# Second products of token tiles 1 and 3 one pair behind those of tiles 0 and 2 in a windowed mix, ELU and MLP kernel

## The chip, the cores and the metric

One core of one Trainium2 chip. The metric is the device time of one execution in microseconds, the median of several runs; beside it stands one profiled execution, from which all rows come. TensorE's granted clock is 1.0 at 2.4 GHz and 0.5 at 1.2 GHz.

## The reference

```python
w = softmax(weight_gen, axis=-1)            # (4, 4096, 8 heads, 7 taps)
x_unf = x_pad[:, idx, :].reshape(B, S, 7, 8, 24)
mixed = np.einsum('bshk,bskhg->bshg', w, x_unf)    # causal window of 7 tokens, d_model 192
h = mixed.reshape(16384, 192) @ w_in               # d_ff 2048
g = np.where(h > 0.0, h, np.exp(np.minimum(h, 0.0)) - 1.0)
out = g @ w_out                                    # (16384, 192)
```

The lines are the reference's in a shortened form; the softmax adds 1e-9 to its sum. All data is fp32.

## The kernel before, in words

Each of the 128 partitions holds a run of 128 consecutive tokens. A **block** is 4 tokens of each partition, that is 4 **token tiles** of 128 tokens, 512 tokens in all; there are 32 blocks. For each block:

- GpSimd makes the mix: `products` (L451, seven taps at once), `pair_sums` (L458), `last_sums` (L464, the last of them writes `mixed`), and for the softmax of a later block `shifted`, `guarded` and `scaled`. VectorE does the softmax's `max`, `sum` and `rec` (L553), ScalarE its exponential.
- VectorE turns `mixed` in 32x32 pieces (`turn`, L778); SP's queue sends it to DRAM and back as `x_raw`; ScalarE rounds it to `xt` (`high_parts`, L630) and GpSimd subtracts for `xt_lo` (`low_parts`, L485). This is done a block ahead.
- The matrix products run on fp32r values in high and low parts. d_ff is cut into 16 chunks, in 8 **pairs**. For a pair TensorE makes the **first products** (`half_products`, L866: high by high, low by high, high by low, 36 matmuls of 64 rows and 512 columns, two halves side by side) into two PSUM slots of four, then the **second products** of the pair before it in four steps (`second_products`, L878). A step takes two of the four accumulators (one PSUM bank for each token tile), half of the rows into one and half into the other: tiles (0, 2), (1, 3), (2, 0), (3, 1). Each step has 4 high matmuls of 384 columns (`g_hi` by `w_out` high and low together) and 4 low ones of 192 columns (`g_lo`).
- Between them lies the ELU: ScalarE `em = exp(h)` and `em - 1`, VectorE `max(min(em, 0), h)` back into the slot (L807), ScalarE `g_hi` (L658), VectorE `g_lo = slot - g_hi` (L813). That is the plain form, for pairs 0 to 3. Pairs 4 to 7 (`low_first`) treat the second chunk first and otherwise: VectorE `min(h, 0)` (L796), ScalarE exp, VectorE add -1 and max (L801). That is one operation fewer on ScalarE and one more on VectorE; it is called the longer form here.

All order is written out by hand: each engine's program is a list of pairs with waits on semaphores, and each engine works strictly in its order. TensorE's order is: first products of pair m + 1, second products of pair m; in pair 7 the first products are those of the next block's pair 0. At the start of a block VectorE must empty the four accumulators of the block before (`outputs`, L786, one reduction over high and low for each tile, in the order 2, 0, 3, 1) before TensorE may start the second products of pair 0 in them; `s_out` counts these reductions, `s_row` the halves of steps that TensorE has done, `s_split` the `g_lo`, `s_ghi` the `g_hi`. The four buffers for `g_hi` and `g_lo` hold two pairs.

```python
                for step, (j, products) in enumerate(steps):
                    if m == 0 and step < 2:
                        ge(pe, s_out, b.count(TILES, 2 * step + 2 - TILES))
                    ge(pe, s_row, b.count(STEPS, 2 * TILES * m + 2 * step - 2))
```

In block 0 the weights are also split: ScalarE rounds a quarter of `w_in` or `w_out` (`hi_half`, L596), VectorE subtracts (`low_half`, L750; its line is L756 where it reads a copy in PSUM, L760 where both inputs are in SBUF). Five of the eight quarters are done between the pairs, by `SPLIT_AT`: behind pair 0 `out` 1, pair 1 `in` 2, pair 2 `out` 2, pair 3 `in` 3, pair 4 `out` 3. They are called the first to the fifth split. `turn` stands ahead of pair 4 in block 0, of pair 3 in block 1, of pair 2 in all others.

## Time and profile before

| what | before |
|---|---|
| median of 3 runs | 1230.33 us (1230.3 to 1230.64) |
| profiled execution, its time | 1231.57 us |
| its span, first to last instruction | 1229.7 us |
| granted TensorE clock, mean | 0.991 |
| busy: TensorE, VectorE, ScalarE, GpSimd | 93%, 75%, 73%, 65% |
| DMA engines, mean over the span | 72 GB/s |

The profiled execution's own time is 1.87 us above its span; differences in the span are compared with that execution. In a timeline row stand the start and the length in us, the engine, the line, the operation with the tile that it writes and those that it reads, how many of them are merged into the row, and in brackets the idle time ahead of it with what ended that. PE is TensorE, PEld its weight loads, DVE VectorE, ACT ScalarE, POOL GpSimd. TensorE's merged rows overlap a little, so starts are compared with starts.

### The profile page before, as it was taken

The page shows a single profiled execution, that of the slowest core. Times are in us where ns is not written, and L with a number is a line of the kernel's source. Part 1 is how long each engine was busy: PE and PEld are TensorE (multiplying, and loading weights), DVE is VectorE, ACT ScalarE, POOL GpSimd, SP SyncE. Part 2 cuts the span into 40 slices and gives each one's busy share as a digit, 9 for nine tenths or more (in the row PEclk, how much of TensorE's full clock was granted, in tenths as well). Part 3 has the DMA queues.
Part 4 walks back from the last instruction along what each step waited for, and adds up shares of the span by engine and source line. Part 5 has one row for each costly group of instructions (what it writes and reads, how often), then busy time and mean ns, then how long its engine had stood idle before and what let it go on. Part 6 is the DMA issues. An engine that isn't in the chain of part 4 may idle for free.

```text
span 1229.7 us, 32008 instructions
## 1 busy us (share of the span) xinstructions
PE 1146.7 (93%) x12848; PEld 1021.8 (83%) x12848; DVE 921.1 (75%) x1431; ACT 900.0 (73%) x1549; POOL 802.4 (65%) x355
## 2 busy tenths in 40 slices
PE   4589999999999999999999999999999999999998
PEld 4478888888888888888888888888888888988887
DVE  7957777777777777777777777777777777777776
ACT  4457777777777777777777777777777777777775
POOL 7775667866667876667876667776667776667410
PEclk9889999999999999999999999999999999999999
DMA  7121333211232211223211233211323311331100
GB/s 217 44 74 40 89 88 88 86 55 33 87 87 87 84 57 33 87 87 87 87 56 31 87 87 87 87 59 30 87 87 87 87 60 31 83 87 51 52 14 14
DMA packets 58774, 88.02 MB, mean 72 GB/s; under 512 B 5224, under 2 KB 38500, under 8 KB 58720
## 3 DMA queue, kind: packets, MB, share of 16 engines
q1 hardware_dynamic: 58720, 87.42, 24.9%
q8 instruction: 19, 0.31, 0.1%
q14 instruction: 35, 0.29, 0.1%
HBM read 62.63 MB, written 24.77 MB: 71 GB/s over the span
## 4 chain that ended last, share of the span: by engine, by line
PE 78%; DVE 10%; ACT 5%; issue 5%; POOL 2%; DMA 0%; DVEq 0%; SPq 0%; POOLq 0%
PE acc L897 40%; PE slot L873 37%; DVE outs L789 5%; DVE g_lo L813 3%; ACT em L642 3%; ACT em L652 2%; POOL prod L453 1%; DMA xwin<-in_x_dram 0%; DVE slot L807 0%; DVE win_lo L760 0%; DVE wout L760 0%; POOL xt_lo L489 0%; POOL prod L470 0%; POOL prod L469 0%; DVE acc L730 0%
## 5 line engine op out<-in xcount | busy, mean ns | idle before, releaser
L897 PE MATMUL acc<-wout,g_hi 64*128 64x384 f32 x4096 | 548.6, 345 | 18.3 <-issue 12.0
L897 PE MATMUL acc<-wout,g_lo 64*128 64x192 f32 x4096 | 380.7, 264 | 44.8 <-DVE g_lo L813 44.4
L897 PEld LDWEIGHTS acc<-wout,g_lo 64*128 64x128 f32 x4096 | 367.0, 186 | 64.0 <-DVE g_lo L813 62.2
L807 DVE SCALAR_TENSOR_TENSOR slot<-em,slot 128x512 f32<-128x512 f32 x384 | 266.3, 695 | 185.9 <-ACT em L652 185.6
L642 ACT ACTIVATE em<-slot 128x512 f32<-128x512 f32 x384 | 227.3, 592 | 205.5 <-PE slot L873 205.5
L897 PEld LDWEIGHTS acc<-wout,g_hi 64*128 64x128 f32 x4096 | 328.7, 188 | 46.0 <-issue 24.4
L489 POOL TENSOR_TENSOR xt_lo<-x_raw,xt 128x512 fp32r<-128x512 f32 x93 | 118.8, 1292 | 358.3 <-ACT xt L635 358.3
L813 DVE TENSOR_TENSOR g_lo<-slot,g_hi 128x512 fp32r<-128x512 f32 x512 | 346.6, 689 | 5.3
L658 ACT ACTIVATE g_hi<-slot 128x512 fp32r<-128x512 f32 x512 | 304.8, 595 | 59.8 <-DVE slot L807 33.9
L453 POOL TENSOR_TENSOR prod<-xwin,probs 128x5376 f32<-128x5376 f32 (+1 forms) x32 | 305.9, 9559 | 7.1 <-POOL probs L448 5.4
L652 ACT ACTIVATE em<-em 128x512 f32<-128x512 f32 x384 | 242.7, 632 | 12.2
L873 PE MATMUL slot<-xt,win_hi 64*128 64x512 f32 (+1 forms) x1548 | 227.3, 399 | 2.6 <-ACT xt L592 1.3
L873 PE MATMUL slot<-xt,win_lo 64*128 64x512 f32 (+1 forms) x1548 | 221.6, 391 | 0.0
L873 PE MATMUL slot<-xt_lo,win_hi 64*128 64x512 f32 (+1 forms) x1548 | 217.8, 386 | 0.0
L873 PEld LDWEIGHTS slot<-xt,win_lo 64*128 64x128 f32 x1548 | 146.3, 186 | 33.6
L873 PEld LDWEIGHTS slot<-xt_lo,win_hi 64*128 64x128 f32 x1548 | 146.0, 186 | 32.2
L461 POOL TENSOR_TENSOR prod<-prod 128x2304 f32<-128x2304 f32 (+1 forms) x32 | 163.6, 5112 | 0.1
L801 DVE SCALAR_TENSOR_TENSOR slot<-em,slot 128x512 f32<-128x512 f32 x128 | 89.1, 696 | 89.8 <-ACT em L647 89.8
L873 PEld LDWEIGHTS slot<-xt,win_hi 64*128 64x128 f32 x1548 | 127.4, 188 | 14.4 <-POOL xt_lo L489 1.4
L647 ACT ACTIVATE em<-em 128x512 f32<-128x512 f32 x128 | 80.9, 632 | 32.3 <-DVE em L796 32.3
L796 DVE TENSOR_SCALAR em<-slot 128x512 f32<-128x512 f32 x128 | 88.5, 691 | 11.7 <-PE slot L873 10.4
L789 DVE TENSOR_REDUCE outs<-acc 128x192 f32<-128x384 f32 x128 | 62.2, 548 | 1.8 <-PE acc L897 1.8
(54 smaller groups left out, 406.2 us busy)
## 6 DMA issues: line engine op xcount, KB each, us to landing
xwin<-in_x_dram SPq DMA_DIRECT2D x29, 960.0 KB, 5.0
x_raw<-turned_dram SPq DMA_DIRECT2D x62, 384.0 KB, 4.7
out_dram<-outs SPq DMA_DIRECT2D x32, 384.0 KB, 2.6
turned_dram<-turned SPq DMA_DIRECT2D x124, 96.0 KB, 2.0
wg<-in_weight_gen_dram SPq DMA_DIRECT2D x32, 112.0 KB, 2.5
xwin<-in_x_dram SPq DMA_DIRECT2D x2, 768.0 KB, 4.6
win_raw<-in_moe_w_in_dram SPq DMA_DIRECT2D x24, 64.0 KB, 3.2
wout_raw<-in_moe_w_out_dram SPq DMA_DIRECT2D x4, 384.0 KB, 4.1
```

The lines of the kernel that those rows point to most:

```text
L453: done = nc.gpsimd.tensor_tensor(prod_of(first, end), taps_of(q, first, end), weights_of(q, first, end), ALU.mult)
L461: nc.gpsimd.tensor_tensor(prod[:, 0:half, first_tile * d_model:], prod[:, 0:half, first_tile * d_model:], prod[:, half:2 * half, first_til ...
L489: nc.gpsimd.tensor_tensor(by_tile(xt_lo[:, parity, k, :]), by_quad(x_raw[:, k, :]), by_tile(xt[:, parity, k, :].bitcast(F32)), ALU.subtrac ...
L642: nc.scalar.activation(em[:, f % 2, :], slot[slot_of(f)], ACT.Exp).then_inc(s_exp, 1)
L652: nc.scalar.activation(em[:, f % 2, :], em[:, f % 2, :], ACT.Copy, bias=-1.0).then_inc(s_em, 1)
L658: nc.scalar.activation(g_hi[:, f % GBUFS, :], slot[slot_of(f)], ACT.Copy).then_inc(s_ghi, 1)
L789: nc.vector.tensor_reduce(outs[:, parity, t, :], acc[t][:, 0:2 * d_model].rearrange("p (k d) -> p d k", k=2), AX.X, ALU.add).then_inc(s_ou ...
L801: nc.vector.scalar_tensor_tensor(out=slot[slot_of(f)], in0=em[:, 1, :], scalar=-1.0, in1=slot[slot_of(f)], op0=ALU.add, op1=ALU.max).then_ ...
L807: nc.vector.scalar_tensor_tensor(out=slot[slot_of(f)], in0=em[:, f % 2, :], scalar=0.0, in1=slot[slot_of(f)], op0=ALU.min, op1=ALU.max).th ...
L813: nc.vector.tensor_tensor(g_lo[:, f % GBUFS, :], slot[slot_of(f)], g_hi[:, f % GBUFS, :].bitcast(F32), ALU.subtract).then_inc(s_split, 1)
L873: last = pe.matmul(slot[slot_of(2 * m + h)][:, tokens], w[rows, k, cols], v[rows, parity, k, tokens], start=(n == 0), stop=(n == PASSES - 1))
L897: last = pe.matmul(acc[t][:, cols], g[rows, f % GBUFS, chunk(t)], wout[rows, f, 0:cols.stop - cols.start], start=(f == 0 and g is g_hi and ...
```

## The change

1. TensorE's second products are taken apart into tile pairs `EVEN` (tiles 0 and 2) and `ODD` (tiles 1 and 3). In the place of pair m's second products stand now: first odd step of pair m - 1, first even step of pair m, second odd step of pair m - 1, second even step of pair m. In pair 0 the pair before is pair 7 of the block before; the odd steps of the very last pair stand behind everything.
2. The outputs come in two groups: tiles 2 and 0 in pair 0 between its `max` and `g_lo`; tile 3 behind the first `max` of pair 1 and tile 1 behind the second. TensorE waits for the first group ahead of the first even step of pair 0 and for the second ahead of the first odd step that clears accumulators 1 and 3, in the place of pair 1.
3. Pair 0 gets the longer form. A `g_hi` buffer is free with the third step behind its pair instead of its own last.
4. TensorE waits for `xt` and `xt_lo` piece by piece instead of for all of `xt_lo`.
5. In blocks 0 and 1: `products` of block 1 are 8 instructions and its `pair_sums` 4; each of the five splits stands on VectorE ahead of the next pair instead of behind its own; `turn` in block 0 stands ahead of pair 5 instead of 4; steps of the softmaxes move by one or more pairs, and the `rec` for block 3 from pair 0 of block 1 to pair 3.

```diff
-    LOWS = PAIRS // 2
+    LOWS = PAIRS // 2 + 1
...
-            return block.count(STEPS, 2 * TILES * done)
+            return block.count(STEPS, 2 * TILES * done + 2)
...
-            return m >= PAIRS // 2
+            return m == 0 or m >= PAIRS // 2
...
+        LAST_ROW = {t: BLOCKS * STEPS - n for t, n in {2: 5, 0: 4, 3: 1, 1: 0}.items()}
...
-        DONE = (2, 0, 3, 1)
+        EVEN = ((0, 2), (2, 0))
+        ODD = ((1, 3), (3, 1))
+
+        def finished(b, t):
+
+            return b.count(STEPS, {2: STEPS - 5, 0: STEPS - 4, 3: STEPS + 1, 1: STEPS + 2}[t] - STEPS)
...
-            def pair_sums(b, first_tile=0):
+            def pair_sums(b, first_tile=0, pieces=1):
 
                 pool.wait_ge(s_prod, b.count(1, 1))
-                nc.gpsimd.tensor_tensor(prod[:, 0:half, first_tile * d_model:], prod[:, 0:half, first_tile * d_model:],
-                                        prod[:, half:2 * half, first_tile * d_model:], ALU.add).then_inc(s_add, 1)
+                each = (TILES - first_tile) // pieces * d_model
+                for at in range(first_tile * d_model, TILES * d_model, each):
+                    done = nc.gpsimd.tensor_tensor(prod[:, 0:half, at:at + each], prod[:, 0:half, at:at + each],
+                                                   prod[:, half:2 * half, at:at + each], ALU.add)
+                done.then_inc(s_add, 1)
...
-            products(1, 0, TILES)
+            for t in range(TILES):
+                for taps in ((0, BANK_TAPS), (BANK_TAPS, kernel)):
+                    done = nc.gpsimd.tensor_tensor(prod_of(t, t + 1)[:, taps[0]:taps[1]], taps_of(1, t, t + 1, taps),
+                                                   weights_of(1, t, t + 1, taps), ALU.mult)
+            done.then_inc(s_prod, 1)
...
-                return {("max", 0): 2, ("exp", 1): 2, ("sum", 1): 2, ("rec", 3): 2,
-                        ("max", 5): 3, ("exp", 7): 3, ("sum", 7): 3}
-            late = 6 if b.has_old else 7
+                return {("max", 0): 2, ("exp", 2): 2, ("sum", 2): 2, ("rec", 4): 2, ("max", 6): 3}
+            late = 7 if number(b) == 1 else 6
             at = {("rec", 0): 2, ("max", 4): 3, ("exp", late): 3, ("sum", late): 3}
+            if number(b) == 1:
+                at = {("exp", 0): 2, ("sum", 1): 2, ("rec", 3): 2, ("max", 4): 3, ("exp", late): 3, ("sum", late): 3}
...
                     softmax_step("rec", m)
-                    if m == turn_at(b)[0] and b.has_next:
+                    if b.first and m - 1 in SPLIT_AT:
+                        low_half(*SPLIT_AT[m - 1])
+                    if m == turn_at(b) and b.has_next:
                         turn(b)
...
                         elu(b, one)
+                        if m == 0 and b.has_previous:
+
+                            dve.wait_ge(s_stored[1 - q], b.per_parity(16, 16 * q))
+                            output(b, 2, 1 - q)
+                            output(b, 0, 1 - q)
                         low(b, two)
                         low(b, one)
                     else:
                         elu(b, one)
+                        if m == 1 and b.has_previous:
+                            output(b, 3, 1 - q)
                         elu(b, two)
-                        if m == 0 and b.has_previous:
-
-                            dve.wait_ge(s_stored[1 - q], b.per_parity(16, 16 * q))
-                            outputs(b, 1, 1 - q)
+                        if m == 1 and b.has_previous:
+                            output(b, 1, 1 - q)
                         low(b, one)
                         low(b, two)
-                    if b.first and m in SPLIT_AT:
-                        low_half(*SPLIT_AT[m])
...
+                rows = 2 * TILES * m - TILES
+                if m == 0 and b.first:
+                    pe.wait_ge(s_ghi, 2)
+                    tiles_of(b, 0, EVEN[0], 0)
+                    tiles_of(b, 0, EVEN[1], 2)
+                    return
+                earlier = (b, m - 1) if m > 0 else (previous(b), PAIRS - 1)
+                if m == 1:
+
+                    ge(pe, s_out, b.count(TILES))
+                tiles_of(*earlier, ODD[0], b.count(STEPS, rows - 2))
+                if m == 0:
+                    pe.wait_ge(s_out, b.count(TILES, 2 - TILES))
+                pe.wait_ge(s_ghi, b.count(CHUNKS, 2 * m + 2))
+                tiles_of(b, m, EVEN[0], b.count(STEPS, rows))
+                tiles_of(*earlier, ODD[1], b.count(STEPS, rows + 2))
+                tiles_of(b, m, EVEN[1], b.count(STEPS, rows + 4))
```

VectorE at the start of a block (any but the first two), before: the two `max` of pair 0, the reductions, two `g_lo`, then pair 1.

```order
L566 RECIPROCAL wrec<-wsum 128x32 [waits s_psoft]
L807 SCALAR_TENSOR_TENSOR slot<-em,slot 128x512 [waits s_em] x2
L789 TENSOR_REDUCE outs<-acc 128x192 [waits s_row,s_stored1]
L789 TENSOR_REDUCE outs<-acc 128x192 [waits s_row] x3
L813 TENSOR_TENSOR g_lo<-slot,g_hi 128x512 [waits s_ghi] x2
L807 SCALAR_TENSOR_TENSOR slot<-em,slot 128x512 [waits s_em] x2
L813 TENSOR_TENSOR g_lo<-slot,g_hi 128x512 [waits s_ghi] x2
```

The same place now:

```order
L589 RECIPROCAL wrec<-wsum 128x32 [waits s_psoft]
L818 TENSOR_SCALAR em<-slot 128x512 [waits s_filled]
L823 SCALAR_TENSOR_TENSOR slot<-em,slot 128x512 [waits s_exp]
L829 SCALAR_TENSOR_TENSOR slot<-em,slot 128x512 [waits s_em]
L811 TENSOR_REDUCE outs<-acc 128x192 [waits s_row,s_stored1]
L811 TENSOR_REDUCE outs<-acc 128x192 [waits s_row]
L835 TENSOR_TENSOR g_lo<-slot,g_hi 128x512 [waits s_ghi] x2
L829 SCALAR_TENSOR_TENSOR slot<-em,slot 128x512 [waits s_em]
L811 TENSOR_REDUCE outs<-acc 128x192 [waits s_row]
L829 SCALAR_TENSOR_TENSOR slot<-em,slot 128x512 [waits s_em]
L811 TENSOR_REDUCE outs<-acc 128x192 [waits s_row]
L835 TENSOR_TENSOR g_lo<-slot,g_hi 128x512 [waits s_ghi] x2
```

Two reductions are ahead of the first two `g_lo` where four were, one operation (L818) came into pair 0, and the other two reductions stand in pair 1.

VectorE in block 0, before, from the end of pair 2 to L796 of pair 5; L760 are the third, fourth and fifth split:

```order
L760 TENSOR_TENSOR wout<-wout_raw,wout 128x4x192 [waits s_whi]
L566 RECIPROCAL wrec<-wsum 128x32 [waits s_psoft]
L807 SCALAR_TENSOR_TENSOR slot<-em,slot 128x512 [waits s_em] x2
L813 TENSOR_TENSOR g_lo<-slot,g_hi 128x512 [waits s_ghi] x2
L760 TENSOR_TENSOR win_lo<-win_raw,win_hi 128x3x256 [waits s_whi]
L783 STREAM_TRANSPOSE turned<-mixed 128x768 [waits s_add]
L796 TENSOR_SCALAR em<-slot 128x512 [waits s_filled]
L801 SCALAR_TENSOR_TENSOR slot<-em,slot 128x512 [waits s_exp]
L807 SCALAR_TENSOR_TENSOR slot<-em,slot 128x512 [waits s_em]
L813 TENSOR_TENSOR g_lo<-slot,g_hi 128x512 [waits s_ghi] x2
L760 TENSOR_TENSOR wout<-wout_raw,wout 128x4x192 [waits s_whi]
L796 TENSOR_SCALAR em<-slot 128x512 [waits s_filled]
```

The same place now:

```order
L585 TENSOR_REDUCE wsum<-probs 128x32 [waits s_esoft]
L782 TENSOR_TENSOR wout<-wout_raw,wout 128x4x192 [waits s_whi]
L829 SCALAR_TENSOR_TENSOR slot<-em,slot 128x512 [waits s_em] x2
L835 TENSOR_TENSOR g_lo<-slot,g_hi 128x512 [waits s_ghi] x2
L589 RECIPROCAL wrec<-wsum 128x32 [waits s_psoft]
L782 TENSOR_TENSOR win_lo<-win_raw,win_hi 128x3x256 [waits s_whi]
L818 TENSOR_SCALAR em<-slot 128x512 [waits s_filled]
L823 SCALAR_TENSOR_TENSOR slot<-em,slot 128x512 [waits s_exp]
L829 SCALAR_TENSOR_TENSOR slot<-em,slot 128x512 [waits s_em]
L835 TENSOR_TENSOR g_lo<-slot,g_hi 128x512 [waits s_ghi] x2
L782 TENSOR_TENSOR wout<-wout_raw,wout 128x4x192 [waits s_whi]
L805 STREAM_TRANSPOSE turned<-mixed 128x768 [waits s_add]
```

`turn` (the transpose) was ahead of pair 4 and is now ahead of pair 5, behind the fifth split; `rec` went from pair 3 to pair 4, `wsum` from pair 1 to the end of pair 2.

## Rows read from the trace of the kernel before

**Rows 1.** The page, part 1: busy time and share of each engine.

```profile
PE 1146.7 (93%) x12848; PEld 1021.8 (83%) x12848; DVE 921.1 (75%) x1431; ACT 900.0 (73%) x1549; POOL 802.4 (65%) x355
```

**Rows 2.** Waits from 119.97 to 1188.5: us in total, times, longest.

```profile
PE acc L897 <- DVE g_lo L813: 41.5, 29, 1.5
```

**Rows 3.** Timeline of TensorE around a block's start: start us, us, line, operation.

```profile
594.67 0.88 PE L873 MATMUL slot<-xt,win_hi 64*128 64x512 f32 x6
...
599.03 0.88 PE L873 MATMUL slot<-xt,win_hi 64*128 64x512 f32 x6
...
601.16 0.62 PE L897 MATMUL acc<-wout,g_hi 64*128 64x384 f32 x4
603.21 0.47 PE L897 MATMUL acc<-wout,g_lo 64*128 64x192 f32 x4 [1.43 <-DVE g_lo L813]
```

**Rows 4.** Timeline of VectorE at the same place.

```profile
600.01 1.94 DVE L789 TENSOR_REDUCE outs<-acc 128x192 f32<-128x384 f32 x4
601.88 1.28 DVE L813 TENSOR_TENSOR g_lo<-slot,g_hi 128x512 fp32r<-128x512 f32 x2
...
605.74 0.97 DVE L783 STREAM_TRANSPOSE turned<-mixed 128x768 f32<-128x768 f32 x1
```

**Rows 5.** Timeline of ScalarE and VectorE in a pair of the longer form.

```profile
1214.68 0.60 ACT L642 ACTIVATE em<-slot 128x512 f32<-128x512 f32 x1 [0.94 <-PE slot L873]
...
1216.83 1.26 ACT L658 ACTIVATE g_hi<-slot 128x512 fp32r<-128x512 f32 x2
...
1217.46 1.36 DVE L813 TENSOR_TENSOR g_lo<-slot,g_hi 128x512 fp32r<-128x512 f32 x2
```

**Rows 6.** Timeline of ScalarE, then of VectorE, in pair 0.

```profile
596.97 0.60 ACT L642 ACTIVATE em<-slot 128x512 f32<-128x512 f32 x1 [0.94 <-PE slot L873]
...
598.26 0.70 DVE L807 SCALAR_TENSOR_TENSOR slot<-em,slot 128x512 f32<-128x512 f32 x1 [1.26 <-ACT em L652]
599.41 0.69 DVE L807 SCALAR_TENSOR_TENSOR slot<-em,slot 128x512 f32<-128x512 f32 x1 [0.45 <-ACT em L652]
```

**Rows 7.** Timeline of VectorE, then of GpSimd, in block 0.

```profile
26.66 3.73 DVE L760 TENSOR_TENSOR wout<-wout_raw,wout 128x768 fp32r<-128x768 f32 x1
...
45.13 10.19 DVE L760 TENSOR_TENSOR win_lo<-win_raw,win_hi 128x768 fp32r<-128x768 f32 x1
...
60.23 0.96 DVE L760 TENSOR_TENSOR wout<-wout_raw,wout 128x768 fp32r<-128x768 f32 x1
61.10 0.68 DVE L796 TENSOR_SCALAR em<-slot 128x512 f32<-128x512 f32 x1
...
31.31 5.15 POOL L461 TENSOR_TENSOR prod<-prod 128x2304 f32<-128x2304 f32 x1
...
39.63 1.84 POOL L470 TENSOR_TENSOR prod<-prod 128x768 f32<-128x768 f32 x1
...
44.79 9.70 POOL L453 TENSOR_TENSOR prod<-xwin,probs 128x5376 f32<-128x5376 f32 x1 [0.27 <-POOL probs L448]
```

**Rows 8.** Timeline of three engines around block 1, and one window.

```profile
69.33 1.66 ACT L635 ACTIVATE xt<-x_raw 128x512 fp32r<-128x512 f32 x3
...
79.72 0.36 DVE L566 RECIPROCAL wrec<-wsum 128x32 f32<-128x32 f32 x1 [4.54 <-POOL wsum L441]
...
78.29 0.88 PE L873 MATMUL slot<-xt,win_hi 64*128 64x512 f32 x6
...
119.97 0.88 PE L873 MATMUL slot<-xt,win_hi 64*128 64x512 f32 x6
...
core 0: us, PE busy (x) PEld busy (x) DVE busy (x) ACT busy (x) POOL busy (x), PEclk, DMA share, GB/s
78.30:92.00 13.70, 10.51 (x82) 8.80 (x80) 7.07 (x13) 5.35 (x10) 13.38 (x7) 0.75 0.32 110
```

**Rows 9.** Timeline at the end: VectorE and TensorE.

```profile
1224.95 1.95 DVE L789 TENSOR_REDUCE outs<-acc 128x192 f32<-128x384 f32 x4 [1.77 <-PE acc L897]
1225.06 0.36 PE L897 MATMUL acc<-wout,g_lo 64*128 64x192 f32 x4
```

More of the change, by code:

```diff
@@ L243, in turn_at, with copies_at @@
         def turn_at(b):
-            return (4, (0, 3)) if b.first else (3, (0, 3)) if not b.has_old and b.pair == 0 else (2, (1, 2))
+            return 5 if b.first else 3 if number(b) == 1 else 2
+        def copies_at(b):
+            return {6: (0, PIECES)} if b.first else {5: (0, PIECES)} if number(b) == 1 else {4: (0, 1), 5: (1, PIECES)}
+        LAST_ROW = {t: BLOCKS * STEPS - n for t, n in {2: 5, 0: 4, 3: 1, 1: 0}.items()}
         def by_quad(t):
@@ L277, in taps_of, with weights_of @@
                            ap=[list(t.ap[0]), [d_model, taps[1] - taps[0]], [group, (end - first) * heads], [1, group]])
[L279 to L280 removed]
+        def weights_of(q, first, end, taps=(0, kernel)):
+            t = probs[:, q, first * HK + taps[0]:]
             return bass.AP(tensor=t.tensor, offset=t.offset,
[L282 removed]
+                           ap=[list(t.ap[0]), [1, taps[1] - taps[0]], [kernel, (end - first) * heads], [0, group]])
         def bank_weights(taps):
@@ L411, in _, with previous @@
                 sp.wait_ge(s_stored[q], 16 * (BLOCKS // 2 + 1))
+        def previous(b):
+            return Block(b.pair, 0) if b.parity == 1 else Block(b.pair - 1, 1)
         def following(b):
@@ L542, in body @@
                 sums(b)
-            sums(one_)
+            sums(one_, pieces=TILES)
             with pool.Fori(1, BLOCKS // 2 - 2) as pair:
@@ L656, in high @@
                 act.wait_ge(s_g, place(b, f))
-                ge(act, s_row, used_count(b, f - GBUFS))
+                if not (b.first and f < GBUFS):
+                    act.wait_ge(s_row, used_count(b, f - GBUFS))
                 nc.scalar.activation(g_hi[:, f % GBUFS, :], slot[slot_of(f)], ACT.Copy).then_inc(s_ghi, 1)
             def body(b):
-                at, pieces = turn_at(b)
                 softmax = softmaxes(b)
@@ L850, in _ @@
             unrolled_blocks(body)
-            b = Block(BLOCKS // 2 - 1, 1)
             dve.wait_ge(s_stored[1], 16 * (BLOCKS // 2))
-            outputs(b, 0, 1)
+            for t in (2, 0, 3, 1):
+                nc.vector.wait_ge(s_row, LAST_ROW[t])
+                nc.vector.tensor_reduce(outs[:, 1, t, :],
+                                        acc[t][:, 0:2 * d_model].rearrange("p (k d) -> p d k", k=2), AX.X,
+                                        ALU.add).then_inc(s_out, 1)
         @block_of.tensor
@@ L871, in half_products @@
                     w, v = ((win_hi, xt), (win_lo, xt), (win_hi, xt_lo))[n // PIECES]
+                    if m == 0 and copied is not None and n // PIECES == 0:
+                        pe.wait_ge(s_xthi, copied.count(PIECES, k + 1))
+                    if m == 0 and copied is not None and n // PIECES == 2:
+                        pe.wait_ge(s_xtlo, copied.count(PIECES, k + 1))
                     for h, rows in enumerate(HALVES):
@@ L882, in second_products @@
                 lo = (g_lo, slice(d_model, 2 * d_model))
-                highs, lows_ = ((one, hi), (two, hi)), ((one, lo), (two, lo))
-                steps = [(j, highs + lows_) for j in range(TILES)]
-                pe.wait_ge(s_ghi, b.count(CHUNKS, two + 1))
-                for step, (j, products) in enumerate(steps):
-                    if m == 0 and step < 2:
-                        ge(pe, s_out, b.count(TILES, 2 * step + 2 - TILES))
-                    ge(pe, s_row, b.count(STEPS, 2 * TILES * m + 2 * step - 2))
-                    for n, (f, (g, cols)) in enumerate(products):
-                        if j == 0 and f == one and g is g_lo:
-                            pe.wait_ge(s_split, b.count(CHUNKS, two + 1))
-                        for h, rows in enumerate(HALVES):
-                            t = (j + 2 * h) % TILES
-                            last = pe.matmul(acc[t][:, cols], g[rows, f % GBUFS, chunk(t)],
-                                             wout[rows, f, 0:cols.stop - cols.start],
-                                             start=(f == 0 and g is g_hi and step < 2),
-                                             stop=(f == CHUNKS - 1 and g is g_lo and j >= 2))
-                            if n == len(products) - 1:
-                                last.then_inc(s_row, 1)
@@ new lines, in tiles_of @@
+                ge(pe, s_row, rows_done)
+                for n, (f, (g, cols)) in enumerate(((one, hi), (two, hi), (one, lo), (two, lo))):
+                    if n == 2 and tiles == EVEN[0]:
+                        pe.wait_ge(s_split, b.count(CHUNKS, two + 1))
+                    for t, rows in zip(tiles, HALVES):
+                        last = pe.matmul(acc[t][:, cols], g[rows, f % GBUFS, chunk(t)],
+                                         wout[rows, f, 0:cols.stop - cols.start],
+                                         start=(f == 0 and g is g_hi and tiles in (EVEN[0], ODD[0])),
+                                         stop=(f == CHUNKS - 1 and g is g_lo and tiles in (EVEN[1], ODD[1])))
+                        if n == 3:
+                            last.then_inc(s_row, 1)
```

37 lines of the change are left out of this document (17 added, 20 removed).

## The prediction

> **What bounds the kernel now.** I read the page first. The reader is to see TensorE busy for 93% of the span and no other engine above 75% [rows 1], so the question is where TensorE stands still. The list of waits answers for the 29 blocks from 120 to 1188.5 us: one wait counts there, 29 times for VectorE's `g_lo`, 41.5 us in all, 1.43 us a block [rows 2]. The timeline of TensorE at a block's start then shows the place [rows 3]. First products of a pair start at 594.67 and of the next at 599.03: a pair costs 4.36 us where nothing waits, of which the first products take 2.10 and the four steps of the second ones 2.26 (0.57 each). Eight pairs are 34.88 us. But a block takes (599.03 - 119.97) / 13 = 36.85 us [rows 3, 8], so 1.97 us are lost per block: 1.43 in that wait, the rest in the restart around it (0.28 before 601.16) and one later pair. VectorE's rows give the reason [rows 4]: from 600.01 it reduces all four accumulators (0.49 us each, start to start), and only then subtracts the two `g_lo`, 601.88 to 603.16; TensorE's low products start at 603.21.
>
> Below, T is the start of the first products of pair 1 (599.03), and F the moment when a pair's two slots are full; at a block's start F = T - 2.08 (ScalarE's exponential, 596.97, starts 0.02 after F [rows 6]).
>
> **The change, part by part.**
>
> *TensorE's order.* No product is added or removed in a block. In the second products of pair 0 TensorE now first does a step of the pair before, so the first `g_lo` is wanted later: 2.10 (first products) + 0.57 (odd step) + 0.35 (high part) = T + 3.02, instead of T + 2.45.
>
> *VectorE and ScalarE in pair 0.* It now takes the form of pairs 4 to 7. VectorE gets one operation more (0.69 us), ScalarE one fewer (0.63). Such a pair, measured: slots full at 1214.66, the two `g_lo` start at 1217.46 when the second `max` ends, so F + 2.80, and end 1.35 later [rows 5]. With two reductions (2 x 0.485 = 0.97) between: F + 5.12 = T + 3.04, and 0.04 to reach TensorE: T + 3.08. Against T + 3.02 a wait of 0.06 is left, and a product that starts after a wait costs 0.11 more than in the stream (0.47 against 0.36 us [rows 3]). I take **0.17 us left per block, so 1.80 saved**. Bounds: 1.97 (nothing left) and 1.2 (VectorE comes 0.6 late to pair 0).
>
> *Pair 1.* The plain form: `max` of the first chunk starts at F + 1.32 and of the second at F + 2.47 [rows 6]. F is T + 2.10. Tile 3 is finished by the third step of pair 0, T + 2.1 + 1.7 + some 0.2 = T + 4.0 to 4.1; VectorE is ready for it at T + 4.1. Then reduction, `max`, reduction, two `g_lo`: T + 7.2. TensorE wants them at T + 6.46 + 0.57 + 0.35 = T + 7.38, and the cleared accumulators at T + 6.46, when VectorE is done with them at T + 5.8. Nothing waits; the slack is 0.2.
>
> *Behind it.* `turn` starts at T + 7.15 in place of T + 6.71 [rows 4]. Its two transfers and ScalarE's first copy, at T + 18.6, have 1.7 us of slack left. On SP's queue the store of the outputs, and the loads of weights and of the window behind it, go out some 3 us later, but are wanted 15 us later at the earliest. A g_hi buffer is now free with the third step of the following pair, F + 1.7 to 1.9; ScalarE asks for it at F + 2.17 [rows 5]. All this costs nothing; the cover is 0.3 us in the last case.
>
> *The start, blocks 0 and 1.* VectorE's splitting of weights (both inputs in SBUF) takes 0.96 us at 60.23, but 3.73 and 10.19 at 26.66 and 45.13 [rows 7]. The second ends 0.8 us after GpSimd's products, 44.79 + 9.70 [rows 7]: while GpSimd runs one long instruction, this operation waits. Now the products and first sums of block 1 are in 12 pieces (a quarter of 5.15 is 1.3, an eighth of the products 1.0 to 1.4), the splits stand one place later, and `turn` behind the last of them.
>
> Followed with these durations, VectorE: pair 0 (now of the longer form) through at 22.1 + 4.15 = 26.2; first split waits for a piece, through near 28.1 instead of 30.4; pair 1 until 30.8; second split 32.2; pair 2 and the `wsum` behind it 36.3; third split, behind a piece, 38.2; pair 3 until 40.9 instead of 45.1; fourth split behind one of the last sums (1.84 [rows 7]), 43.7; pair 4 (4.15), 47.8. GpSimd: products 19.9 to 31.1 (8 pieces, a split between them), first sums with two splits between until 38.9, `wsum` 0.3, three sums of 1.84 and a split 6.5, scaling 0.8: products of block 2 from 46.4 to 56.1 instead of 44.8 to 54.5. So the fourth split, which waited 9.2 us, goes free, but VectorE comes to the fifth at 47.8, 1.4 us after those products began, and it waits until 57. `turn` follows, pair 5 begins at 57.9 instead of 61.10 [rows 7]: 3.2 us gained, but `turn` ends at 57.9 instead of 56.2. ScalarE copied x 13.1 us after `turn`'s end, when its pair 6 was through [rows 8]; the data needs 9.1 (last transfer issued at 60.9, landing 4.4 to 4.7 later), so the copies now start at 67.0, the last `xt_lo` is there at 71.5, pair 7 at 72.7. The first products of block 1 no longer wait for the last `xt_lo`: T of block 1 comes at about 74.2 instead of 78.29 [rows 8], **4.1 us**. In block 1 before, VectorE stood 4.54 us for GpSimd's `wsum` [rows 8], TensorE's granted clock was 0.75 over the 13.7 us behind (1.2 GHz for half of them), and the block took 119.97 - 78.29 = 41.68. `rec` has moved to pair 3, so block 1 should take 34.88 + 0.5 (pair 0) + 1.2 (`turn` in pair 3 waits for `mixed`) = 36.6: **5.1 us**. Together 9.2. Bounds: 5 (the pieces give nothing) and 18 (the last split comes before the products).
>
> The Trainium skill (SBUF — State Buffer, Who interferes with whom) says that a VectorE instruction with two SBUF inputs and a GpSimd one that reads SBUF block each other for a whole instruction, and that issue order decides who waits. The long split's row agrees on the first; no row here shows the order between two ready pieces. Read literally it speaks against this part, since GpSimd's next piece could be issued ahead of the split; the sum would then be 1171.6 (rival C).
>
> *The end.* TensorE has one odd step more behind the last wait (0.57) and a step that waits for the one before it (some 0.2). Four reductions from 1224.95, the first beside the last products of 1225.06 [rows 9], become two behind the end, which saves some 0.4: **0.4 us more**.
>
> **Sum**, against the profiled execution (span 1229.7, time 1231.57): 30 boundaries (into blocks 2 to 31) x 1.80 = 54.0; start 9.2; end -0.4: 62.8 us less, a span of 1166.9. The median of the runs is 1230.33, and the same difference gives **1167.5 us**.
>
> **Rivals.**
> (A) The forecast, its range 1160 to 1176, chance 0.62.
> (B) The boundary wait shrinks but stays: VectorE has the longer chain in pair 0, and any lateness goes one for one into TensorE's wait. For it: the margin is nil (-0.06). Against: VectorE ends a pair 0.2 before the next F (1218.82 against 1219.02 [rows 5]), and `rec` takes 0.34 of which only 0.05 is late. With 0.6 more per block: 18 us, 1185. Chance 0.14.
> (C) GpSimd's pieces let no split in until its queue waits for a semaphore. For it: its rows stand back to back, and no row shows a split between two ready pieces. Then the first 4.1 are lost: 1171.6. Chance 0.13. The page of the Trainium skill named above would have it so if its order of issue is that of the queues.
> (D) VectorE reaches the last split before the products of block 2 start; it is only 1.4 us late by my working. It then saves 8 of the 9.2 us that it waits: 1159. Chance 0.07.
> (E) Slower: each step of the second products waits for its accumulators' last step. If the new interleaving made it wait for the step directly ahead of it, as at the end, each of 1024 steps would pay a restart of 0.11 to 0.2 us. From 0.06 us per step that eats the gain of 62.8; at 0.11 it costs 113 us: 1280. Against: the counts waited for lie two steps back in both orders, and consecutive steps always use other banks. Chance 0.03.
> (F) The wait does not go because something else, late at the same place, ends it: no change but the start's. I give no change within 0.2% (about what a measurement of this kernel can tell) 0.01.
>
> **How the numbers follow.** The likeliest is A: 1167.5. The range 1158 to 1184 takes in A, C, D and most of B's bounds. Faster: A to D, 0.96; same 0.01; slower 0.03.
>
> **What would show it.** In the new profile TensorE's wait for `g_lo` at the low product should be under 0.2 us per block and the block period 35.0 to 35.1; VectorE's reductions should stand in two pairs, with a `max` between the later two and the first `g_lo` pair ending near T + 3.1. The last split should show some 9 us, the other splits under 2.5. Block 1's T near 74, block 2's near 111, with no stretch at a granted clock of 0.75 behind 78. A period above 35.4 would refute the pair-0 working, a T of block 1 above 77 the start's.

## The result, and the profile after

The changed kernel took 1159.7 us in the median of its first four runs, against 1230.32 for the kernel before in the same comparison: a ratio of 0.943, with a 95% interval of 0.9376 to 0.9484. The four runs were 1155.2, 1155.6, 1163.8 and 1165.6; two later sets gave 1165.2 (four runs, ratio 0.9469, 0.9455 to 0.9484) and 1166.1 (five runs, ratio 0.9474, 0.9461 to 0.9487). The forecast was 1167.5. So there are two groups of runs, near 1155 (two runs) and from 1163.8 to 1167.3 (eleven); the first median, 1159.7, lies between them, where no run does, and what follows on the profile is about the longer group. The profiled execution took 1163.79 us with a span of 1162.0, 67.7 less than before.

The page of the changed kernel: TensorE's busy share and the granted clock in 40 slices.

```profile
PE 1129.5 (97%) x12848; PEld 1027.8 (88%) x12848; DVE 926.4 (80%) x1463; ACT 882.1 (76%) x1517; POOL 806.5 (69%) x365
...
PEclk9989999999999999999999999999999999999999
```

TensorE is busy for 97% of the span instead of 93% [rows 1]. In the list of waits from 110 to 1115 us (us in total, times, longest) the line that answers to [rows 2]:

```profile
PE acc L922 <- DVE g_lo L835: 0.4, 1, 0.4
```

The wait that counted 29 times is left once, in block 2. TensorE at the block's start that answers to [rows 3]:

```profile
598.91 0.88 PE L907 MATMUL slot<-xt,win_hi 64*128 64x512 f32 x6
...
601.55 0.53 PE L922 MATMUL acc<-wout,g_hi 64*128 64x384 f32 x4
601.92 0.36 PE L922 MATMUL acc<-wout,g_lo 64*128 64x192 f32 x4
...
603.27 0.88 PE L907 MATMUL slot<-xt,win_hi 64*128 64x512 f32 x6
```

T is 598.91. From T to the next first products are 4.36 us, as between any two pairs: the low product of 601.92 runs 0.37 behind the high one, 0.36 long, so nothing was waited for. VectorE in pairs 0 and 1 of the same block, answering to [rows 4, 6]:

```profile
596.88 0.69 DVE L818 TENSOR_SCALAR em<-slot 128x512 f32<-128x512 f32 x1
...
598.93 0.69 DVE L829 SCALAR_TENSOR_TENSOR slot<-em,slot 128x512 f32<-128x512 f32 x1
599.54 1.01 DVE L811 TENSOR_REDUCE outs<-acc 128x192 f32<-128x384 f32 x2
600.47 1.27 DVE L835 TENSOR_TENSOR g_lo<-slot,g_hi 128x512 fp32r<-128x512 f32 x2
...
603.11 0.55 DVE L811 TENSOR_REDUCE outs<-acc 128x192 f32<-128x384 f32 x1
603.65 0.70 DVE L829 SCALAR_TENSOR_TENSOR slot<-em,slot 128x512 f32<-128x512 f32 x1
604.25 0.55 DVE L811 TENSOR_REDUCE outs<-acc 128x192 f32<-128x384 f32 x1
604.72 1.28 DVE L835 TENSOR_TENSOR g_lo<-slot,g_hi 128x512 fp32r<-128x512 f32 x2
605.92 0.97 DVE L805 STREAM_TRANSPOSE turned<-mixed 128x768 f32<-128x768 f32 x1
```

Two reductions from 599.54, `g_lo` until 601.74, which is 0.18 before TensorE's low product; then a reduction on each side of the second `max` of pair 1 (603.65), and the transpose at T + 7.01. The span splits as follows; the T of blocks 1, 2 and 31 are starts of TensorE's first products:

```profile
73.13 0.88 PE L907 MATMUL slot<-xt,win_hi 64*128 64x512 f32 x6
...
108.93 0.88 PE L907 MATMUL slot<-xt,win_hi 64*128 64x512 f32 x6
...
1122.35 0.88 PE L907 MATMUL slot<-xt,win_hi 64*128 64x512 f32 x6
```

| stretch | before | after | difference | forecast |
|---|---|---|---|---|
| start to T of block 1 | 78.29 | 73.13 | -5.2 | -4.1 |
| block 1 | 41.68 | 35.80 | -5.9 | -5.1 |
| blocks 2 to 30 | 1068.6 | 1013.4 | -55.2 | -52.2 |
| block 31, to the last exponential | 30.4 | 28.5 | -2.0 | -1.8 |
| from there to the end | 10.7 | 11.2 | +0.5 | +0.4 |
| span | 1229.7 | 1162.0 | -67.7 | -62.8 |

The starts of 1188.6 and 1219.04 (before) and 1150.82 (after) come from the same timelines. VectorE and GpSimd in block 0, where L782 are the splits, answering to [rows 7]:

```profile
26.41 1.20 DVE L782 TENSOR_TENSOR wout<-wout_raw,wout 128x768 fp32r<-128x768 f32 x1
...
36.39 1.49 DVE L782 TENSOR_TENSOR wout<-wout_raw,wout 128x768 fp32r<-128x768 f32 x1
...
40.62 1.81 DVE L782 TENSOR_TENSOR win_lo<-win_raw,win_hi 128x768 fp32r<-128x768 f32 x1
...
46.49 8.98 DVE L782 TENSOR_TENSOR wout<-wout_raw,wout 128x768 fp32r<-128x768 f32 x1
55.39 0.96 DVE L805 STREAM_TRANSPOSE turned<-mixed 128x768 f32<-128x768 f32 x1
...
18.76 11.41 POOL L533 TENSOR_TENSOR prod<-xwin,probs 128x768 f32<-128x768 f32 x8
...
25.59 1.21 POOL L533 TENSOR_TENSOR prod<-xwin,probs 128x576 f32<-128x576 f32 x1
26.75 2.26 POOL L533 TENSOR_TENSOR prod<-xwin,probs 128x768 f32<-128x768 f32 x1
...
44.95 9.71 POOL L469 TENSOR_TENSOR prod<-xwin,probs 128x5376 f32<-128x5376 f32 x1 [0.27 <-POOL probs L464]
```

The rows of 25.59 and 26.75 are the sixth and seventh of the eight pieces in the row above them, taken by a narrower window. The first split, started at 26.41, took 1.20 us: it ended 0.81 behind the sixth piece, and the seventh took 2.26 us where its like took 1.54, so it was the seventh that waited. GpSimd's program has no wait between these pieces. The third split (1.49) got in between the last piece of the first sums and `wsum`, the fourth (1.81) waited for the second half of one of the last sums and went ahead of the next. The fifth was reached at 46.49, 1.5 us after the products of block 2 began, and took 8.98: it ended 0.8 behind them. TensorE's rows, and then a window, show what that costs, answering to [rows 8]:

```profile
59.67 1.01 PE L922 MATMUL acc<-wout,g_hi 64*128 64x384 f32 x4 [8.91 <-ACT g_hi L683]
...
63.07 1.42 PE L907 MATMUL slot<-xt,win_hi 64*128 64x512 f32 x6
```

```profile
core 0: us, PE busy (x) PEld busy (x) DVE busy (x) ACT busy (x) POOL busy (x), PEclk, DMA share, GB/s
50.00:73.00 23.00, 13.57 (x132) 12.10 (x132) 17.55 (x20) 11.44 (x20) 10.97 (x6) 0.78 0.22 52
```

TensorE stood 8.91 us and came back at 1.2 GHz: the six products at 63.07 take 1.42 us instead of 0.88; over the window the granted clock is 0.78. The stretch at 0.75 behind 78 is gone, as forecast: from 78 to 92 us the granted clock is 1.00. At T of block 2 stand VectorE's `rec` and two of TensorE's rows with what is left of the waits:

```profile
107.94 0.35 DVE L589 RECIPROCAL wrec<-wsum 128x32 f32<-128x32 f32 x1 [0.70 <-POOL wsum L457]
...
112.06 0.61 PE L922 MATMUL acc<-wout,g_hi 64*128 64x384 f32 x4 [0.32 <-DVE outs L811]
113.07 0.47 PE L922 MATMUL acc<-wout,g_lo 64*128 64x192 f32 x4 [0.40 <-DVE g_lo L835]
```

The end, answering to [rows 9]: TensorE's last odd step, and VectorE's last reductions, of which now only two stand behind it.

```profile
1157.27 0.62 PE L922 MATMUL acc<-wout,g_hi 64*128 64x384 f32 x4
...
1156.72 1.02 DVE L881 TENSOR_REDUCE outs<-acc 128x192 f32<-128x384 f32 x2 [1.76 <-PE acc L922]
1158.13 1.02 DVE L881 TENSOR_REDUCE outs<-acc 128x192 f32<-128x384 f32 x2 [0.39 <-PE acc L922]
```

### The profile page after: what moved, and what is told of

It is laid out like the page before. It is cut to its first block, busy times and chain, and to the rows that moved or that the text cites. A ratio compares the mean times of both kernels' runs of the same rounds, so it can differ in the third digit from the quotient of the medians.

```text
span 1162.0 us, 32004 instructions
## 1 busy us (share of the span) xinstructions
PE 1129.5 (97%) x12848; PEld 1027.8 (88%) x12848; DVE 926.4 (80%) x1463; ACT 882.1 (76%) x1517; POOL 806.5 (69%) x365
## 4 chain that ended last, share of the span: by engine, by line
PE 86%; POOL 7%; issue 2%; DVE 2%; DMA 1%; ACT 1%; SPq 0%; POOLq 0%; DVEq 0%
PE acc L922 45%; PE slot L907 42%; POOL prod L469 2%; POOL prod L479 2%; POOL prod L533 1%; DVE g_lo L835 1%; POOL xt_lo L508 1%; DMA turned_dram<-turned 0%; DMA x_raw<-turned_dram 0%; POOL prod L488 0%; POOL prod L489 0%; DVE slot L823 0%; DVE slot L829 0%; ACT em L671 0%; DVE outs L811 0%
## 5 line engine op out<-in xcount | busy, mean ns | idle before, releaser
L922 PE MATMUL acc<-wout,g_lo 64*128 64x192 f32 x4096 | 374.3, 260 | 0.8 <-DVE g_lo L835 0.4
L922 PEld LDWEIGHTS acc<-wout,g_lo 64*128 64x128 f32 x4096 | 371.0, 185 | 4.7 <-DVE g_lo L835 3.4
L666 ACT ACTIVATE em<-slot 128x512 f32<-128x512 f32 x352 | 208.5, 592 | 133.6 <-PE slot L907 133.6
L469 POOL TENSOR_TENSOR prod<-xwin,probs 128x5376 f32<-128x5376 f32 (+1 forms) x31 | 296.4, 9561 | 7.2 <-POOL probs L464 6.8
L676 ACT ACTIVATE em<-em 128x512 f32<-128x512 f32 x352 | 222.7, 633 | 11.2
L479 POOL TENSOR_TENSOR prod<-prod 128x2304 f32<-128x2304 f32 (+2 forms) x35 | 164.8, 4711 | 0.1
L818 DVE TENSOR_SCALAR em<-slot 128x512 f32<-128x512 f32 x160 | 109.4, 684 | 8.1 <-PE slot L907 7.9
L659 ACT ACTIVATE xt<-x_raw 128x512 fp32r<-128x512 f32 x93 | 54.8, 625 | 23.3 <-DMA x_raw<-turned_dram 23.1
```

The costliest lines, as they stand in the source:

```text
L469: done = nc.gpsimd.tensor_tensor(prod_of(first, end), taps_of(q, first, end), weights_of(q, first, end), ALU.mult)
L479: done = nc.gpsimd.tensor_tensor(prod[:, 0:half, at:at + each], prod[:, 0:half, at:at + each], prod[:, half:2 * half, at:at + each], ALU.add)
L666: nc.scalar.activation(em[:, f % 2, :], slot[slot_of(f)], ACT.Exp).then_inc(s_exp, 1)
L676: nc.scalar.activation(em[:, f % 2, :], em[:, f % 2, :], ACT.Copy, bias=-1.0).then_inc(s_em, 1)
L818: nc.vector.tensor_scalar_min(em[:, 1, :], slot[slot_of(f)], 0.0).then_inc(s_low, 1)
L922: last = pe.matmul(acc[t][:, cols], g[rows, f % GBUFS, chunk(t)], wout[rows, f, 0:cols.stop - cols.start], start=(f == 0 and g is g_hi and ...
```

## The experiments

T of block 1 and of block 2 and the period of the later blocks (the commonest distance of two T, to within 0.01 or 0.02) are from each kernel's profile. The three profiles of the changed kernel have T of block 1 up to 0.9 us apart, so a smaller difference there says nothing. All kernels ran beside the kernel before, which had medians of 1230.65, 1230.66 and 1231.16 us.

| kernel | median us | T of block 1 | T of block 2 | period |
|---|---|---|---|---|
| before | 1230.3 | 78.29 | 119.97 | 36.85 |
| changed (profiles of three sets) | 1159.7, 1165.2, 1166.1 | 73.13, 73.89, 74.00 | 108.93, 109.72, 109.82 | 34.88 |
| start_only | 1224.9 | 75.23 | 112.07 | 36.85 |
| longform_before | 1225.2 | 79.11 | 121.56 | 36.51 |
| whole | 1167.4 | 76.04 | 111.88 | 34.88 |
| gate | 1157.2 | 65.39 | 101.24 | 34.88 |
| gate_plain0 | 1165.0 | 66.26 | 102.16 | 35.21 |
| gate_extra | 1170.1 | 65.98 | 102.20 | 35.32 |
| gate_strict | 1157.2 | 66.08 | 101.87 | 34.88 |
| whole_x | 1161.6 | 70.17 | 106.00 | 34.88 |
| turn_first | 1156.6 | 64.94 | 100.78 | 34.88 |

**again, again2: the changed kernel, unaltered.**

> The changed kernel, unaltered. Its four runs so far were 1155.2, 1155.6, 1163.8 and 1165.6 us, with mean granted clocks of 0.998, 0.997, 0.993 and 0.992, so there are two groups some 9 us apart. Theory: they are two outcomes of block 0. In one VectorE's fifth split waits 9 us for GpSimd's products of block 2 (as in the profiled run, T of block 1 at 73.1), in the other it starts ahead of them and T comes some 8 us earlier, with no stretch at half clock near 60 us. Rival: the steady part differs, by a lowered clock somewhere behind 110 us. If the profile falls into the fast group, T of block 1 near 65 speaks for the theory, 73 for the rival.

> The changed kernel, unaltered, once more, since of eight runs two were 9 us shorter and no profile of such a run is at hand. Theory: in those VectorE's fifth split started ahead of GpSimd's products of block 2, as the gated kernel (1157.15) makes it do always; a profile in the fast group must then show that split at about 1 us and T of block 1 near 65. Rival: split at 9 us also in a fast profile, with the time gained elsewhere. If all runs are slow (1164 to 1166) it stays open.

All nine runs lay in the longer group: 1164.7 to 1165.6 and 1165.7 to 1167.3. There is no edit. Both profiles show the fifth split at 8.98 us. No profile of a run near 1155 was had, so what happened in the two of 13 stays open. Their mean granted clocks, 0.998 and 0.997, are those of the gated kernel below (0.996 to 0.999) and not those of the other eleven (0.992 to 0.994), which fits a missing stand of TensorE and does not show it; the next experiment shows that a deliberate early split gives about that time.

**gate: GpSimd starts the products of block 2 only when all splits are done.**

```diff
                 pool.wait_ge(s_add, b.count(ADDS))
+                pool.wait_ge(s_wlo, len(SPLITS))
                 products(q, 0, TILES)
```

> The changed kernel; GpSimd's products of block 2 (and of all later blocks, where it costs nothing) also wait until all eight splits are done. Theory (the fifth split's 9 us wait is what sets T of block 1): the split takes about 1 us, TensorE has no idle stretch of 9 us between 50 and 60, T of block 1 near 65 instead of 73.1, all runs in one group at 1153 to 1157 us. Rival (the transfers of x and GpSimd's later products hide it): T of block 1 stays at 71 to 73 and the runs at 1162 to 1166.

1157.15 us (1155.95 to 1157.6), ratio 0.9404 (0.9391 to 0.9417) to the kernel before, and 8.0 less than the changed kernel beside it. VectorE and GpSimd in its timeline, and a window of it:

```profile
46.63 0.96 DVE L783 TENSOR_TENSOR wout<-wout_raw,wout 128x768 fp32r<-128x768 f32 x1
...
47.73 9.73 POOL L469 TENSOR_TENSOR prod<-xwin,probs 128x5376 f32<-128x5376 f32 x1 [2.91 <-DVE wout L783]
```

```profile
50.00:73.00 23.00, 20.58 (x218) 17.00 (x216) 17.25 (x29) 16.53 (x30) 17.04 (x7) 1.00 0.25 61
```

The split takes 0.96 instead of 8.98 and GpSimd starts 2.8 later; the long stand of TensorE is gone and the clock stays at 1.00. T of block 1 is at 65.39, 8.5 earlier than in the changed kernel beside it. The theory of the fifth split holds, and this version is faster than the kernel before and than the longer group of the changed one.

**whole: products and first sums of block 1 as one instruction each.**

```diff
-            for t in range(TILES):
-                for taps in ((0, BANK_TAPS), (BANK_TAPS, kernel)):
...
+            products(1, 0, TILES)
...
-            sums(one_, pieces=TILES)
+            sums(one_)
```

> The changed kernel with products and first sums of block 1 in one instruction each again (12 pieces to 2). Theory: the first and third split wait for the long instructions, 2 to 4 us each, VectorE reaches the fifth split 3 to 5 us later, but that waits for the products of block 2 all the same, so T of block 1 stays within 1.5 us of 73.1: 1162 to 1167 us, and no run in the group near 1155. Rival (the pieces carry the gain at the start): 1168 us or more.

1167.4 against 1165.2 beside it: T of block 1 is 2.0 to 2.9 later. That is more than my 1.5, and the median lies just above my range and just below the rival's. Its VectorE and GpSimd:

```profile
32.27 3.79 DVE L778 TENSOR_TENSOR win_lo<-win_raw,win_hi 128x768 fp32r<-128x768 f32 x1
...
48.79 8.98 DVE L778 TENSOR_TENSOR wout<-wout_raw,wout 128x768 fp32r<-128x768 f32 x1
...
39.40 0.90 POOL L457 TENSOR_TENSOR wsum<-wsum,eps 128x32 f32<-128x32 f32 x1 [4.16 <-DVE wsum L581]
...
47.24 9.71 POOL L469 TENSOR_TENSOR prod<-xwin,probs 128x5376 f32<-128x5376 f32 x1 [0.27 <-POOL probs L464]
```

The first two splits take 3.16 and 3.79 us (I had named the first and third; the third took 0.95), so `wsum` comes late, GpSimd stands 4.16 for it, and the products of block 2 start at 47.24 instead of 44.95. The fifth split waits behind them as before. I had left out that the late splits hold GpSimd up through `wsum`.

**start_only: the start's part alone, on the kernel before.** Its edits are those of the change's fifth item, among them:

```diff
-                    if b.first and m in SPLIT_AT:
-                        low_half(*SPLIT_AT[m])
...
-            products(1, 0, TILES)
+            for t in range(TILES):
+                for taps in ((0, BANK_TAPS), (BANK_TAPS, kernel)):
...
-            sums(one_)
+            sums(one_, pieces=TILES)
```

> The kernel before with the start's part of the change alone (pieces, splits one place later, turn of block 0 at pair 5, softmax steps moved); TensorE's order, outputs and pair 0 as before. By the prediction's sum the start is worth 9.2 us of 62.8; the changed profile says 11.0 with all parts. Theory: 1219 to 1222 us, the block period still 36.85. Rival (the start gains only together with TensorE's new order): 1225 or more.

1224.9 us, 5.7 less, ratio 0.9957 (0.9942 to 0.9973), outside my 1219 to 1222 and just short of the rival. The profiled execution was the shortest of the four (1223.76 to 1225.79): its span is 7.8 less, T of block 2 is 7.9 earlier and the period unchanged. That is less than the 9.2 to 11 of the theory. TensorE's rows show what is missing:

```profile
70.78 0.96 PE L881 MATMUL slot<-xt,win_hi 64*128 64x512 f32 x6 [1.04 <-POOL xt_lo L492]
...
79.41 0.47 PE L905 MATMUL acc<-wout,g_lo 64*128 64x192 f32 x4 [1.46 <-DVE g_lo L821]
```

TensorE stands 1.04 us for all of `xt_lo` ahead of block 1, which the piecewise wait takes away, and the wait at the boundary, 1.46 us here, stays in block 1, which takes 36.84 us instead of 35.80. So the 11 us at the start of the changed kernel are 8 of this part and 3 of the others.

**whole_x: the gated kernel, TensorE waits for all of `xt_lo` again.**

```diff
                     elif b.has_next:
+                        pe.wait_ge(s_xtlo, b.count(PIECES, PIECES))
                         pe.wait_ge(s_split, b.count(CHUNKS, CHUNKS - 2))
-                        half_products(1 - q, 0, range(PASSES), copied=b)
+                        half_products(1 - q, 0, range(PASSES))
```

> The gated kernel in which TensorE again waits for all of xt_lo before the first products of the next block. Theory: in later blocks xt_lo is there long before (period stays 34.9), in block 0 the products start some 3 us later, of which 2.1 us are those that now run ahead of the last xt_lo: T of block 1 near 67.5 and 1159 to 1160 us. Rival (the piecewise wait is worth nothing): 1157.

1161.6 us, 4.4 more, T of block 1 at 70.17. TensorE's row of those products:

```profile
63.58 1.65 PE L908 MATMUL slot<-xt,win_hi 64*128 64x512 f32 x6 [4.91 <-POOL xt_lo L508]
```

They start 4.5 later than in the gated kernel (59.04), behind a stand of 4.91 us, and the first six of them take 1.65 us; the granted clock from 63 to 66 us is 0.50, where the gated kernel has 1.00. All 36 first products ran at half the clock: 4.01 us from 63.58 to the next second products, where they take 2.10 at the full one. The stand also cost the clock, which I had not counted; T of block 1 is 4.8 later and not 2.1. The later blocks do not change.

**turn_first: the gated kernel with `turn` ahead of the fifth split.**

```diff
-                    if b.first and m - 1 in SPLIT_AT:
-                        low_half(*SPLIT_AT[m - 1])
                     if m == turn_at(b) and b.has_next:
                         turn(b)
+                    if b.first and m - 1 in SPLIT_AT:
+                        low_half(*SPLIT_AT[m - 1])
```

> The gated kernel with turn ahead of the fifth split instead of behind it. Theory: in the gated kernel ScalarE's copies of x in block 0 wait 2.5 us for the transfers behind turn; turn ends 0.9 earlier, so do the copies, but GpSimd's products, which wait for the split, end 0.9 later and hold the first xt_lo: T of block 1 0 to 1 us earlier than 65.4, 1156 to 1157 us. Rival (turn alone counts): 1155 or less.

1156.6 us (1155.3 to 1157.4) against 1157.15 in another set: T of block 1 is 0.45 earlier, as the theory has it, but that is less than the 0.9 by which profiles of one kernel differ there, and the medians do not tell the two kernels apart. It stays open; the rival's 1155 or less did not come.

**longform_before: the kernel before with the longer form in pair 0.**

```diff
-            return m >= PAIRS // 2
+            return m == 0 or m >= PAIRS // 2
```

> The kernel before with only the longer form in pair 0 (TensorE's order, outputs and start as before). Theory: the second max of pair 0 ends 0.36 us earlier (F + 2.80 instead of F + 3.16), the four reductions and g_lo follow, so the wait for g_lo falls from 1.43 to about 1.1 us and the block period from 36.85 to 36.5: 30 x 0.36 = 11 us, 1219 to 1221 us. Rival (VectorE's added operation eats it): 1230 or more.

The period falls by 0.35 to 36.51, as computed; TensorE's wait there:

```profile
601.41 0.47 PE L897 MATMUL acc<-wout,g_lo 64*128 64x192 f32 x4 [1.22 <-DVE g_lo L813]
```

But the median is 1225.2, 5.5 less and not 11: T of block 3 comes 2.1 us later than before (158.90 against 156.84), so the first blocks give part of it back: block 0 0.8, block 1 0.8, block 2 0.5. In block 1 VectorE's `rec` stands 4.53 us for GpSimd's `wsum`, as before. Now L796 stands behind it and ScalarE's exponential waits for L796, so TensorE stands 3.11 us for `g_hi` in that block instead of 1.73.

**gate_plain0: the gated kernel with pair 0 in the plain form.** The first two reductions then stand behind its second `max`.

```diff
-            return m == 0 or m >= PAIRS // 2
+            return m >= PAIRS // 2
```

> The gated kernel (1157.15) with pair 0 in the plain form again. In the changed profile g_lo ends 2.83 us after T and is wanted at T + 3.01, so the slack is 0.18. Theory: the reductions and g_lo come 0.36 later, a wait of about 0.2 and a restart of 0.1 come back: block period 35.1 to 35.3, 1164 to 1170 us. Rival (TensorE's new order alone takes the wait away): period 34.88, 1157 us.

1165.0 us, period 35.21: 0.33 per block come back, and with them 7.9 us (the mean of blocks 2 to 30 is 35.22 instead of 34.94, 8.0 us in all). So, since start_only left the period where it was, whole_x did not change it and gate_strict shows the buffers' release to be free, TensorE's new order with outputs in two groups is worth 36.85 - 35.21 = 1.64 us per block and the longer form 0.33. The order and the two groups were not run apart.

**gate_extra: one more reduction in pair 0.**

```diff
+                            dve.wait_ge(s_row, finished(b, 2))
+                            nc.vector.tensor_reduce(spare[:], acc[2][:, 0:2 * d_model].rearrange("p (k d) -> p d k", k=2),
+                                                    AX.X, ALU.add)
                             output(b, 2, 1 - q)
```

> The gated kernel with one more reduction (into a spare tile) ahead of the two in pair 0 of every block but the first. Theory (the chain of VectorE in pair 0 has 0.18 us of slack and every further us goes into TensorE's wait): 0.485 - 0.18 + 0.1 = 0.4 us per block, period 35.3, 31 x 0.4 = 12.5 us: 1168 to 1171 us. Rival (more slack than the rows show, or a wait for something else): below 1160.

1170.1 us, period 35.32, 0.44 more. VectorE and TensorE at a block's start:

```profile
598.80 0.55 DVE L864 TENSOR_REDUCE spare<-acc 128x192 f32<-128x384 f32 x1
599.27 1.01 DVE L813 TENSOR_REDUCE outs<-acc 128x192 f32<-128x384 f32 x2
600.20 1.28 DVE L837 TENSOR_TENSOR g_lo<-slot,g_hi 128x512 fp32r<-128x512 f32 x2
...
601.53 0.47 PE L927 MATMUL acc<-wout,g_lo 64*128 64x192 f32 x4 [0.18 <-DVE g_lo L837]
```

The wait is back, 0.18 us idle and a product of 0.47 instead of 0.36. `g_lo` ends at 601.48 and the product starts at 601.53, so of the 0.18 us between `g_lo` and the product in the changed kernel 0.05 are the way to TensorE and 0.13 are slack. My estimates with 0.13 come out at both ends: 0.485 - 0.13 + 0.11 = 0.46 here (measured 0.44) and 0.36 - 0.13 + 0.11 = 0.34 in gate_plain0 (measured 0.33). The chain of VectorE in pair 0 is the next limit.

**gate_strict: g_hi buffers free a step later.**

```diff
-            return block.count(STEPS, 2 * TILES * done + 2)
+            return block.count(STEPS, 2 * TILES * done + 4)
```

> The gated kernel in which ScalarE waits for a g_hi buffer until the fourth instead of the third step behind its pair. The third step ends at about F + 1.9 and ScalarE asks at F + 2.17 (cover 0.3), the fourth at F + 2.45. Theory: g_hi comes up to 0.3 us later in pairs of the longer form, but TensorE wants it only at F + 4.9 and g_lo at F + 5.3 (they come at F + 3.4 and 4.2): period 34.9, 1157 to 1158 us. Rival (the buffers' release is the next limit): 0.3 per pair, 8 pairs, 31 blocks: over 1200 us.

1157.2 us, period 34.88. Its waits (whole run):

```profile
ACT g_hi L684 <- PE acc L923: 34.2, 123, 1.0
...
PE acc L923 <- DVE g_lo L836: 0.6, 2, 0.4
```

ScalarE now waits 34.2 us in 123 places (in the gated kernel 0.4 in one), and the period does not show it.

## Why the prediction was right

*The wait at the block's start: right, its rest too large.* I had the pair's `g_lo` end at F + 5.12, 0.06 us too late, and left 0.17 per block. It ends at F + 4.92 (601.74, with F at 596.82), 0.18 ahead of its product, and in most blocks nothing is left: they take 34.88. The mean of blocks 2 to 30 is 34.95, with block 2 at 36.08; without it 34.91. The term that was mis-sized is "F + 5.12", 0.20 too much. I began the reductions where the second `max` ends, but they start 0.08 before that (599.54, with the `max` from 598.93 for 0.69); I took 0.97 for two reductions, but `g_lo` starts 0.93 behind the first (600.47); and the two `g_lo` take 1.27 behind a reduction instead of 1.35 behind a `max`. The rows of the kernel before had it: reductions at 600.01 under a `max` that ends at 600.10 [rows 4, 6] and 1.28 for the two `g_lo` behind them [rows 4]. Blocks 3 to 30 gave 4.1 us more than forecast and block 2 took 1.0 back, so 3 of the 4.9 us between forecast and measured span lie here. gate_extra and gate_plain0 bear out the margin; rival B, a wait that shrinks but stays, is what those two kernels have, and single blocks of the changed one (last section).

*Pair 1 and behind: right.* The reductions stand on both sides of the `max`, `turn` at T + 7.01 (forecast 7.15), and the buffers cost nothing even when made stricter (gate_strict).

*The start: the right places, all 1 to 1.5 us early.* Forecast were the fifth split at 47.8 with 9 us, the products of block 2 from 46.4, T of block 1 at 74.2; measured 46.49 with 8.98, 44.95 and 73.13. The clock stretch behind 78 went with VectorE's stand for `wsum`, as forecast. Rival C (no split gets in between two ready pieces) falls by the rows of 26.41 and 26.75; behind the third and fourth split GpSimd's next instruction has a wait in the program, so those two do not decide it. The Trainium skill (SBUF — State Buffer, Who interferes with whom) lets issue order decide who waits; here the VectorE instruction that waited from 26.41 was let in ahead of GpSimd's next piece, which started at 26.75 and had nothing to wait for in its program. That agrees with the rule if the order of issue is that of the rows' starts, and not if it is that of the queues. Rival D (the last split ahead of the products) was priced at 8 us: the gated kernel, which forces it, gives 8.0. The pieces, which were meant to free the splits, are worth 2.2 us (whole).

*What I did not have:* block 2 loses 1.2 us (108.93 to 145.01), where `rec` waits 0.70 for `wsum` and TensorE 0.32 and 0.40 behind it, since GpSimd is late out of block 1. There it now stands itself:

```profile
80.59 0.26 POOL L457 TENSOR_TENSOR wsum<-wsum,eps 128x32 f32<-128x32 f32 x1 [4.44 <-DVE wsum L585]
```

Moving the softmax steps has turned VectorE's stand of 4.54 us for GpSimd into one of 4.44 us of GpSimd for VectorE. That block 2 pays for it is my reading of these rows; no run varied it. And two of 13 runs were 9 us shorter, outside the 1158 of the range; a forecast for one outcome of block 0 cannot hold both. That the first set's median, 1159.7, lies inside the range is the chance of two runs of each kind; the later sets, 1165.2 and 1166.1, are the ones to hold against 1167.5.

*Rival E* (each step waits for the one ahead of it) falls by the pair of 4.36 us, unchanged.

## What to carry to other kernels

Where one engine's chain between two stages is longer than the work that covers it, look for work of the earlier stage that can be moved behind the boundary: moving half of the second products by one pair gave the chain 0.57 us of cover and took half of the reductions (0.97 us) out of it, together 1.64 us per block as measured, where a shorter chain alone gave 0.35. Add up such chains from start to start, in rows with the same neighbours, not from durations: `g_lo` came 0.18 ahead of its product, and my sum had it 0.06 late. And where a short VectorE operation with both inputs in SBUF can meet a long GpSimd instruction, order the two by a wait: it cost GpSimd 2.8 us and gave 8.
